# One level of Strassen's algorithm in a three-stage fused kernel: seven products of half blocks in place of eight, over chunks of 768 tokens

## The chip, the cores and the metric

The kernel runs on one core of one Trainium2 chip. The metric is device microseconds of one execution. The engines named below are PE (TensorE, matrix products), DVE (VectorE), ACT (ScalarE), POOL (GpSimd) and SP (SyncE, which here only issues DMAs). Each works through its own list of instructions in order and waits for others by counting semaphores.

## The reference, cut to what matters

Three stages follow each other, with fixed sizes: batch 4, 8 heads, 576 positions, head width 64; so 2304 tokens of width 512.

```python
# stage 0: two attentions per head, added (one on positions averaged by 4, one over |i-j| < 4)
x = (up(sm_attn(q_d, k_d, v_d)) + local_attn(q, k, v))      # 2304 x 512
# stage 1
xn = x / sqrt(mean(x*x) + 1e-6) * rms_g
y  = (silu(xn @ w_gate) * (xn @ w_val)) @ w_out             # 512 -> 1536 -> 512
# stage 2
h  = x @ w_in ; r = maximum(h, 0) ; out = (r*r) @ w_out     # 512 -> 2048 -> 512
```

Stage 1 has three matrix products (gate, value, output), stage 2 has two ("first" and "second").

## The kernel before, in words

**Precision.** Every matrix product of stages 1 and 2 is done in three passes of a 4-byte format (fp32r): each operand is split into a high part (a rounded copy, made on ACT) and a low part (the rest, a subtraction on DVE or POOL), and high x high, low x high and high x low are added in PSUM (`PASSES`). So one product of a 128-row weight block costs three matmuls per 128 rows of contraction.

**Stage 0** is 52 units `g` of attention (four groups of 13: nine "local" and four "down" units). For each unit PE forms scores (`qk`), DVE takes maxima, subtracts and sums, ACT takes exponents, POOL multiplies by the reciprocal sums (`normalise`), PE transposes and multiplies by v, ACT copies the output to `xT`, which holds the activations with the width on partitions. PE runs three to four units behind. POOL adds the "down" result at the end of a group (`add_down`). Into this phase other work is put by tables of unit numbers: the split of six weight pieces (`SPLIT_AT`), and for the first token chunk the squares, their sums and the twelve steps of the reciprocal root (`SQUARES_AT`, `SUM_SQ_AT`, `ROOT_AT`). After the last unit DVE normalises the first chunk and splits it (lines 760 and 766), and only then PE starts gate of chunk 0 (line 986).

**Stage 1** goes over six chunks of 384 tokens, and in each over 12 blocks `j` of 128 hidden columns. For each block PE does gate and value (`hidden`, line 986: 12 matmuls with a moving operand of 384 columns each) and the output product (`project`, line 1017: 12 matmuls of 384 columns into four PSUM banks). ACT takes the sigmoid from PSUM (line 540), DVE multiplies by gate and value out of PSUM (795, 798), ACT and DVE split the result (545, 802). The next chunk's mean square, root, normalisation and split are spread over the blocks. The activations `xs` have two buffers.

**Stage 2** goes over six chunks of 384 and 16 blocks `m` of 128: 12 matmuls of 384 columns (line 986 again), relu on ACT (605), square on DVE (840), split (610, 846), and the second product (`project2`, line 1085: 9 matmuls of 512 columns into three banks).

**Weights.** All of stage 1's weights lie split in SBUF: 36 pieces of 128x512, loaded once, with a high half made on ACT (line 495) and a low half on POOL (line 419). Stage 2's pieces take their places as stage 1's last chunk frees them. SP issues those loads in order of pieces (line 364).

PSUM has eight banks: four take the output product, two gate, one value, one the mean square (stage 1); two take the first product and six the second (stage 2). What orders the work is the order written out by hand for each engine. In the profile, lines of helpers are those of the copy `kernel.py`.

Of the kernel before, what the change touches and what calls it, by code (L numbers as in the profile page):

```python
# [48 lines left out]
C1 = 384  # L49
N1 = T // C1  # L50
C2 = 384
N2 = T // C2
TT2 = C2 // 128
PIECE = 512
NPIECE1 = 3 * J1
NPIECE2 = 2 * J2
PA = 6
NRAW = NPIECE1 + NPIECE2
FREE_0, FREE_1 = PA + 9, PA + 13
RING = 4  # L60
GSLOT = NPIECE2
LAG2 = 2
GRING = 4


SPLIT_AT = (21, 24, 27, 30, 35, 38)
SQUARES_AT = (34, 35, 37)
SUM_SQ_AT = (36, 37, 39)
MEAN_SQ_AT = 41
ROOT_AT = (42, 43, 44, 45, 46, 47, 48, 48, 49, 49, 50, 50)  # L70
# [5 lines left out]
ADD_DOWN_AT = (5, 7, 11, 12)  # L76
ADD_DOWN_OF = (0, 2, 1, 3)


def fused_kernel(nc, q_d, k_d, v_d, w1_d, w2_d, rms_d, out_d):  # L80
# [9 lines left out]
    with ctx:  # L90
# [8 lines left out]
        wrawA = [sb(f"wrawA{n}", [128, 2, PIECE], stack=rawA) for n in range(PA)]  # L99
        rawA.close()  # L100
        wsplitA = sb("wsplitA", [128, PA, 2, PIECE], f32r)
        gvec = sb("gvec", [128, KT])
        work = sb("work", [128, TT2 * DM])
        ssq, nrm, tmp = (work[:, C1 * x:C1 * x + C1] for x in range(3))
        ostage = work[:, :].rearrange("p (a b) -> p a b", a=TT2)
        xs0 = sb("xs0", [128, 2, KT, C1], f32r)
        ones = sb("ones", [128, 128])
# [8 lines left out]
        vquad = sb("vquad", [HK, 2, 2, FACTOR, GC], stack=att)  # L116
        qs[1] = sb("qs1", [128, NH, S], stack=att)
        kp[1] = sb("kp1", [128, NH, S + 2 * HALO], stack=att)
        vwin[1] = sb("vwin1", [KW, 2, NL, GC], stack=att)
        vd = sb("vd", [HK, 2, 2, GC], stack=att)  # L120
        qd = sb("qd", [128, NH, SDP], stack=att)
        kd = sb("kd", [128, NH, SD], stack=att)
# [10 lines left out]
        mask = sb("mask", [128, 3, KW], bf16, stack=att)  # L133
        identb = sb("identb", [128, 128], bf16, stack=att)
        ident = sb("ident", [128, 128], stack=att)
        att.close()

        rawB = ExitStack()
        wrawB = [sb(f"wrawB{n}", [128, 2, PIECE], stack=rawB) for n in range(NPIECE1 - PA)]
        rawB.close()  # L140
        wsplitB = sb("wsplitB", [128, NPIECE1 - PA, 2, PIECE], f32r)
        xs = [xs0, sb("xs1", [128, 2, KT, C1], f32r)]
        hb = sb("hb", [128, 2, 2, C1], f32r)
        sig = sb("sig", [128, 2, C1])
        prod = sb("prod", [128, 2, C1])

        def wslot(n):
            return wsplitA[:, n] if n < PA else wsplitB[:, n - PA]

        def wraw(n):  # L150
            return (wrawA[n] if n < PA else wrawB[n - PA])[:, 1, :]

        def slot_of(n):

            return n if n < NPIECE1 else n - NPIECE1

# [4 lines left out]
        ACC, G, V, SS = P[0:4], P[4:6], P[6], P[7]  # L161
        HID, OUT = P[6:8], [P[0:3], P[3:6]]
# [9 lines left out]
        wraw_in = [sem(f"wraw_in{i}") for i in range(RING)]  # L172
# [17 lines left out]
        wh_done, wl_done = sem("wh_done"), sem("wl_done")  # L190

        sq_done, ss_add, ss_mm, nr = sem("sq_done"), sem("ss_add"), sem("ss_mm"), sem("nr")
        xn_done, xh_done, xl_done = sem("xn_done"), sem("xh_done"), sem("xl_done")

        g_done, v_done, o_done = sem("g_done"), sem("v_done"), sem("o_done")
        sig_done, u_done, a_done = sem("sig_done"), sem("u_done"), sem("a_done")
        h_done, l_done = sem("h_done"), sem("l_done")
        y_done = sem("y_done")

        h2_done, o2_done = sem("h2_done"), sem("o2_done")  # L200
        r_done, s_done, gh_done, gl_done = sem("r_done"), sem("s_done"), sem("gh_done"), sem("gl_done")
        zh_done, zl_done = sem("zh_done"), sem("zl_done")
        ev_done = sem("ev_done")
# [8 lines left out]
        def number(eng, n):  # L212

            if not isinstance(n, int):
                eng.compute_val(n)
            return n

        def apart(eng):

            eng.wait_ge(consts, NCONST)  # L220
# [67 lines left out]
        def _(sp):  # L288
# [31 lines left out]

            load_k(0, K_PARTS[0], K_PARTS[1], k_part[0])
# [7 lines left out]
            for b in range(1, NG):  # L329
# [12 lines left out]
                if b == 1:  # L342
                    sp.dma_start(gvec[:, :], rms_d).then_inc(misc_in, 16)
                    for n in range(RING):
                        sp.dma_start(wraw(n), w1_d[n]).then_inc(wraw_in[n], 16)
                if b == 2:
                    for n in range(RING, PA):
                        sp.wait_ge(wh_done, n - RING + 1)
                        sp.dma_start(wraw(n), w1_d[n]).then_inc(wraw_in[n % RING], 16)

            for n in range(PA, NRAW):
                sp.wait_ge(wh_done, n - RING + 1)
                if n == PA:
# [785 lines left out]
```

## Time and profile before

| | |
|---|---|
| median of 3 runs | 1017.39 us (1017.31 to 1018.33) |
| profiled execution, its own time | 1024.89 us |
| its span (first to last instruction) | 1022.9 us |
| PE busy | 989.4 us (97%) |
| DVE, ACT, POOL busy | 423.8, 322.0, 162.9 us |
| mean granted TensorE clock | 0.973 of 2.4 GHz |

"PE" are matmuls and "PEld" the loads of their stationary operand; each matmul has one load. Both are pipelined: a matmul's recorded duration is longer than the distance to the next, so costs are read as distances (a count in a window where PE never idles), not as durations. A row of a group gives lines, engine, operation, tiles, shapes, the count, then busy time and mean ns of one, then the idle time ahead and what ended it.

### The profile page before, as it was taken

Reading aid. Unit: us, or ns where it says so; the run is one execution under the profiler, and the core shown is the slowest. Engines: PE = TensorE matmul, PEld = TensorE weight load, DVE = VectorE, ACT = ScalarE, POOL = GpSimd, SP = SyncE. Lnnn points to the kernel's source line nnn. Section 1 sums busy time; section 2 is a strip of 40 time slices with the busy share of each in tenths; the row PEclk is TensorE's granted clock in tenths of the full one; section 3 lists DMA queues with packets and bytes.
Section 4 is the critical chain, followed back from the end, with each engine's and each line's share of the span. In section 5 each row is a group of like instructions: output and inputs, shape, how many; then the busy total and the mean of one; then the engine's idle time right before and its main releaser. Section 6 shows DMA issues by size and latency. Waiting matters only on the chain.

```text
span 1022.9 us, 16131 instructions
## 1 busy us (share of the span) xinstructions
PE 989.4 (97%) x6404; PEld 918.7 (90%) x6404; DVE 423.8 (41%) x783; ACT 322.0 (31%) x698; POOL 162.9 (16%) x151
## 2 busy tenths in 40 slices
PE   6899959999999999999999999999999999999998
PEld 5677748999999999999999999999999999999997
DVE  6678892543443443443442322323333233332322
ACT  3556554442122122122123333223222222232221
POOL 3356556640000000000002661000000000000000
PEclk9779878999999999999999999999999999999999
DMA  9968302310000000000002440000000000000000
GB/s 241 175 149 211 89 2 93 123 53 1 1 1 1 1 1 1 1 1 1 1 1 64 133 133 2 1 1 32 1 31 1 1 31 1 16 16 1 31 1 31
DMA packets 27972, 42.84 MB, mean 42 GB/s; under 512 B 2300, under 2 KB 14972, under 8 KB 27516
## 3 DMA queue, kind: packets, MB, share of 16 engines
q1 hardware_dynamic: 26316, 40.64, 14.7%
q10 hardware_dynamic: 1584, 1.18, 0.4%
q8 instruction: 52, 0.85, 0.4%
q14 instruction: 20, 0.16, 0.1%
HBM read 37.10 MB, written 4.72 MB: 41 GB/s over the span
## 4 chain that ended last, share of the span: by engine, by line
PE 90%; DVE 5%; issue 3%; DMA 1%; ACT 1%; POOL 1%; SPq 0%; DVEq 0%; ACTq 0%
PE bank L986 49%; PE bank L1085 20%; PE bank L1017 15%; PE bank L922 1%; PE bank L941 1%; PE bank L962 1%; PE bank L916 1%; DVE sml L683 1%; PE bank L937 1%; PE bank L973 1%; DVE mxl L662 1%; DMA kp<-k_dram 1%; DVE qd L705 1%; PE bank L911 0%; PE bank L885 0%
## 5 line engine op out<-in xcount | busy, mean ns | idle before, releaser
L986 PE MATMUL bank<-xs,wsplitB 128*128 128x384 f32 x2376 | 436.8, 335 | 0.0
L986 PEld LDWEIGHTS bank<-xs,wsplitB 128*128 128x128 f32 x2376 | 416.8, 188 | 6.9
L1085 PE MATMUL bank<-wsplitB 128*128 128x512 f32 x702 | 174.4, 393 | 0.0
L1085 PEld LDWEIGHTS bank<-wsplitB 128*128 128x128 f32 x702 | 130.7, 188 | 23.7
L840 DVE TENSOR_TENSOR prod<-sig 128x384 f32<-128x384 f32 x96 | 53.6, 558 | 222.2 <-ACT sig L605 222.2
L1017 PE MATMUL bank<-hb,wsplitB 128*128 128x384 f32 x720 | 136.1, 336 | 1.4 <-ACT hb L545 1.4
L1017 PEld LDWEIGHTS bank<-hb,wsplitB 128*128 128x128 f32 x720 | 125.6, 188 | 3.3 <-POOL wsplitB L419 1.6
L798 DVE TENSOR_TENSOR prod<-prod,bank 128x384 f32<-128x384 f32 x72 | 39.9, 554 | 192.5 <-PE bank L986 192.4
L605 ACT ACTIVATE sig<-bank 128x384 f32<-128x384 f32 x96 | 47.2, 492 | 229.5 <-PE bank L986 229.5
L545 ACT CAST hb<-prod 128x384 fp32r<-128x384 f32 x72 | 37.0, 514 | 248.1 <-DVE prod L798 248.1
L986 PE MATMUL bank<-xs,wsplitA 128*128 128x384 f32 x504 | 96.4, 343 | 3.8 <-DVE xs L766 3.8
L986 PEld LDWEIGHTS bank<-xs,wsplitA 128*128 128x128 f32 x504 | 90.6, 191 | 6.0 <-issue 4.6
L419 POOL TENSOR_TENSOR wsplitB<-wrawB,wsplitB 128x512 fp32r<-128x512 f32 x56 | 72.8, 1327 | 35.3 <-ACT wsplitB L495 35.3
L846 DVE TENSOR_TENSOR wsplitB<-prod,wsplitB 128x384 fp32r<-128x384 f32 x96 | 53.6, 558 | 55.7 <-ACT wsplitB L610 55.7
L419 POOL TENSOR_TENSOR wsplitA<-wrawA,wsplitA 128x512 fp32r<-128x512 f32 x12 | 15.2, 1280 | 334.5 <-ACT wsplitA L495 334.5
L610 ACT CAST wsplitB<-prod 128x384 fp32r<-128x384 f32 x96 | 49.3, 514 | 60.0 <-DVE prod L840 60.0
L802 DVE TENSOR_TENSOR hb<-prod,hb 128x384 fp32r<-128x384 f32 x72 | 41.2, 572 | 42.2 <-ACT hb L545 42.2
L540 ACT ACTIVATE sig<-bank 128x384 f32<-128x384 f32 x72 | 35.5, 492 | 62.8 <-PE bank L986 62.8
L795 DVE TENSOR_TENSOR prod<-sig,bank 128x384 f32<-128x384 f32 x72 | 39.6, 550 | 27.8 <-ACT sig L540 27.8
L1085 PE MATMUL bank<-wsplitA,wsplitB 128*128 128x512 f32 x162 | 40.5, 394 | 0.0
L1085 PEld LDWEIGHTS bank<-wsplitA,wsplitB 128*128 128x128 f32 x162 | 30.2, 188 | 5.5
L962 PEld LDWEIGHTS bank<-probT,vwin 70*64 70x64 f32 x576 | 23.0, 155 | 10.9 <-issue 9.7
(75 smaller groups left out, 746.4 us busy)
## 6 DMA issues: line engine op xcount, KB each, us to landing
wrawB<-w_dram SPq DMA_DIRECT2D x56, 256.0 KB, 3.0
vquad<-v_dram SPq DMA_DIRECT2D x16, 288.0 KB
out_dram<-work SPq DMA_DIRECT2D x18, 256.0 KB, 2.0
kp<-k_dram SPq DMA_DIRECT2D x3, 1152.0 KB, 13.7
qs<-q_dram SPq DMA_DIRECT2D x3, 1152.0 KB, 20.8
vwin<-v_dram SPq DMA_DIRECT2D x6, 512.0 KB
wrawA<-w_dram SPq DMA_DIRECT2D x12, 256.0 KB, 4.7
vwin<-v_dram SPq DMA_DIRECT2D x2, 320.0 KB
```

What stands on the lines that cost most here:

```text
L419: nc.gpsimd.tensor_tensor(wslot(slot)[:, 1], wraw(slot), wslot(slot)[:, 0].bitcast(fp32), ALU.subtract).then_inc(wl_done, 1)
L545: nc.scalar.copy(hb[:, tp, 0, :], prod[:, tp, :]).then_inc(h_done, 1)
L605: nc.scalar.activation(sig[:, tp, 0:C2], HID[tp][:, 0:C2], ACT.Relu).then_inc(r_done, 1)
L610: nc.scalar.copy(wslot(GSLOT + gp)[:, 0, 0:C2], prod[:, tp, 0:C2]).then_inc(gh_done, 1)
L795: nc.vector.tensor_tensor(prod[:, tp, :], sig[:, tp, :], G[tp][:, 0:C1], ALU.mult).then_inc(u_done, 1)
L798: nc.vector.tensor_tensor(prod[:, tp, :], prod[:, tp, :], V[:, 0:C1], ALU.mult).then_inc(a_done, 1)
L802: nc.vector.tensor_tensor(hb[:, tp, 1, :], prod[:, tp, :], hb[:, tp, 0, :].bitcast(fp32), ALU.subtract).then_inc(l_done, 1)
L840: nc.vector.tensor_tensor(prod[:, tp, 0:C2], sig[:, tp, 0:C2], sig[:, tp, 0:C2], ALU.mult).then_inc(s_done, 1)
L846: nc.vector.tensor_tensor(w[:, 1, 0:C2], prod[:, tp, 0:C2], w[:, 0, 0:C2].bitcast(fp32), ALU.subtract).then_inc(gl_done, 1)
L986: last = mm(bank[:, 0:cols], wslot(n)[:, pw, 128 * k:128 * k + 128], x[:, px, k, 0:cols], start=(i == 0 and k == 0), stop=(i == 2 and k == ...
L1017: last = mm(ACC[m][:, 0:C1], wslot(3 * j + 2)[:, pw, 128 * m:128 * m + 128], hb[:, j % 2, px, :], start=(j == 0 and i == 0), stop=(j == J1 ...
L1085: last = mm(OUT[par][tt][:, :], gs[:, px, 128 * tt:128 * tt + 128], w[:, pw, :], start=(m == 0 and i == 0), stop=(m == J2 - 1 and i == 2))
```

## The change

Gate and value (and, in stage 2, the first products of two blocks of 128 columns) are one matrix product of 512 x 256 x 768 per block `u`. Over chunks of 768 tokens this product is cut in two along each of its three sides: contraction (2 x 256), hidden columns (2 x 128; gate and value, or two blocks of stage 2) and tokens (2 x 384). One level of Strassen's algorithm, in Winograd's form, gives the four quarter results from seven products (`NP = 7`) of combined operands instead of eight. Each product is 6 matmuls of 384 columns (`product`). There are 60 units: 3 chunks x 12, then 3 chunks x 8.

- The combined activations (`xcomb`, four sums, `combine_x`) and seven split operands `xs` (single buffer) are made per chunk: 7 copies on ACT (`x_high`) and 7 subtractions on DVE (`x_low`), each 768 elements per partition, and 4 combinations (POOL for the first chunk, DVE for the rest).
- The weights are no longer kept: each unit's four raw quarters are loaded again (4 DMAs of 128 KB), POOL makes four combinations (`combine`), ACT seven high parts (`weights_high`) and POOL five and DVE two low parts (`weights_low`), each 256 elements, one unit ahead, in two slots. Only the output weights stay (`wo`), loaded in order from the end of stage 0 on, behind a wait for all of stage 0.
- The results are summed out of two PSUM banks used in turn (`XY`): per unit ACT copies products 0 and 2 (`first_copy`, `copy_11`), DVE adds products 1, 3, 4, 5, 6 (`add`), each 384 elements.
- Sigmoid, gating and split then work from SBUF on 768 elements. The relu is folded with the square into one DVE instruction per 768 elements (`square`).
- The output product takes 24 matmuls per unit: 12 of 512 columns and 12 of 256 (`project`, 6 banks), cut into segments between the seven products and two units behind (`SEGS`, `LAG_P`). The second product of stage 2 takes 36 matmuls of 512 columns per unit, one unit behind (`SEGS2`).
- In the diff below the loops are, in this order, those of SP, POOL, DVE and PE.
- For the first chunk the mean square is taken with tokens on partitions: twelve root steps on 6 elements each, then spread by a diagonal (`diagonals` on POOL, `spread`), and normalisation and splits go into units 45 to 52 of the attention. For the other two chunks the root steps have 768 elements.

```diff
+HC = 384
+CS = 2 * HC
+U1, U2 = J1, J2 // 2
+BLK = 256
+NP = 7
+CONTINUES = (2, 5, 6)
+HIGH_ORDER = (0, 2, 5, 1, 3, 4, 6)
+POOL_LOW = (0, 2, 5, 1, 3)
+DVE_LOW = (4, 6)
+LAG_P = 2
+SEGS = (3, 3, 4, 3, 4, 3, 4)
+SEGS_FIRST = (0, 0, 4, 5, 5, 5, 5)
+SEGS2 = (0, 0, 5, 7, 8, 8, 8)
...
+        XY = [P[7], P[4]]
+        ACC = P[0:4] + P[5:7]
...
+            for u in range(NUF):
+                if u == 0:
+
+                    sp.wait_ge(oe_done, G_ALL)
                     sp.wait_ge(x_done, ND * NG)
+                    for n in range(3):
+                        load_wo(n)
+                if u < U1 - 3:
+                    load_wo(u + 3)
...
+                if u + 2 < NUF:
+                    load_w(u + 2)
...
+            for u in range(1, NUF - 1):
+                for n in range(4):
+                    combine(u + 1, n)
+                for p in POOL_LOW:
+                    weights_low(u + 1, p)
...
+            ROOT_PLACE = {5: (1, 2), 6: (3, 4, 5), 7: (6, 7, 8), 8: (9, 10, 11)}
+            NORM_PLACE = {9: (0, 1, 2, 3)}
...
+                add(u, 1)
+                if 0 < u <= NU1:
+                    gated(u - 1)
+                    valued(u - 1)
...
+                add(u, 3)
+                if 0 < u <= NU1:
+                    hidden_low(u - 1)
...
+                if normed:
+                    for n in ROOT_PLACE.get(j, ()):
+                        root(c + 1, n)
+                add(u, 4)
+                if prepares:
+                    weights_low(w, DVE_LOW[0])
...
+                if normed:
+                    for k in NORM_PLACE.get(j, ()):
+                        normalise(c + 1, k)
...
+                add(u, 5)
...
+            def product(u, p):
+                low_ready(pe, u, p)
+                if place(u) == 0:
+                    pe.wait_ge(xl_done, NP * chunk_of(u) + p + 1)
+                s = slot0(u) + p
+                bank_free(s)
                 for i, (pw, px) in enumerate(PASSES):
+                    for k in range(2):
+                        last = mm(XY[s % 2][:, 0:HC], wst[:, u % 2, p, pw, 128 * k:128 * k + 128], xs[:, p, px, k, :],
+                                  start=(p not in CONTINUES and i == 0 and k == 0), stop=(i == 2 and k == 1),
+                                  skip_group_check=True)
+                last.then_inc(pr_done, 1)
...
+            for u in range(NUF):
+                for p in range(NP):
+                    if u > 0 or p > 2:
+                        product(u, p)
...
+                    elif LAG_P <= u < NU1:
+                        n1 = n + (SEGS_FIRST if j == 2 else SEGS)[p]
+                        project(u - LAG_P, n, n1)
```

## Rows read from the trace of the kernel before

**Rows 1.** The page, busy time by engine and the span in 40 slices.
```profile
PE 989.4 (97%) x6404; PEld 918.7 (90%) x6404; DVE 423.8 (41%) x783; ACT 322.0 (31%) x698; POOL 162.9 (16%) x151
PEclk9779878999999999999999999999999999999999
GB/s 241 175 149 211 89 2 93 123 53 1 1 1 1 1 1 1 1 1 1 1 1 64 133 133 2 1 1 32 1 31 1 1 31 1 16 16 1 31 1 31
```
**Rows 2.** Chain that ended last, its shares by engine.
```profile
PE 90%; DVE 5%; issue 3%; DMA 1%; ACT 1%; POOL 1%; SPq 0%; DVEq 0%; ACTq 0%
```
**Rows 3.** Windows: stretch: its us, then each engine's busy us (instructions), clock, DMA.
```profile
350.00:450.00 100.00, 100.00 (x576) 99.73 (x575) 41.93 (x79) 21.23 (x43) 0.00 (x0) 1.00 0.00 1
800.00:900.00 100.00, 100.00 (x504) 90.67 (x503) 30.64 (x53) 26.43 (x51) 0.00 (x0) 1.00 0.05 17
120.00:135.00 15.00, 12.37 (x229) 9.85 (x230) 14.62 (x33) 7.35 (x20) 6.43 (x8) 1.00 0.01 3
135.00:147.00 12.00, 6.74 (x88) 5.06 (x86) 11.76 (x21) 6.79 (x23) 8.27 (x5) 0.81 0.01 1
```
**Rows 4.** Groups by line, whole span, PE and its weight loads.
```profile
L986 PE MATMUL bank<-xs,wsplitB 128*128 128x384 f32 x2376 | 436.8, 335 | 0.0
L986 PEld LDWEIGHTS bank<-xs,wsplitB 128*128 128x128 f32 x2376 | 416.8, 188 | 6.9
L1085 PE MATMUL bank<-wsplitB 128*128 128x512 f32 x702 | 174.4, 393 | 0.0
```
**Rows 5.** Timeline, start and length in us: a run of 64-column loads at full clock.
```profile
129.02 0.55 PEld L962 LDWEIGHTS bank<-probT,vwin 70*64 70x64 f32 x16 [0.20 <-issue]
```
**Rows 6.** Groups by line, DVE, 160 to 1022 us.
```profile
L840 DVE TENSOR_TENSOR prod<-sig 128x384 f32<-128x384 f32 x96 | 53.6, 558 | 222.2 <-ACT sig L605 222.2
L795 DVE TENSOR_TENSOR prod<-sig,bank 128x384 f32<-128x384 f32 x72 | 39.6, 550 | 27.8 <-ACT sig L540 27.8
L766 DVE TENSOR_TENSOR xs<-xT,xs 128x768 fp32r<-128x768 f32 x10 | 9.5, 953 | 0.0
```
**Rows 7.** Groups by line, POOL, whole span.
```profile
L419 POOL TENSOR_TENSOR wsplitB<-wrawB,wsplitB 128x512 fp32r<-128x512 f32 x56 | 72.8, 1327 | 35.3 <-ACT wsplitB L495 35.3
```
**Rows 8.** Timeline, DVE beside a busy POOL.
```profile
169.89 10.69 POOL L419 TENSOR_TENSOR wsplitB<-wrawB,wsplitB 128x512 fp32r<-128x512 f32 x8
173.15 0.94 DVE L802 TENSOR_TENSOR hb<-prod,hb 128x384 fp32r<-128x384 f32 x1 [0.95 <-ACT hb L545]
179.81 1.18 DVE L802 TENSOR_TENSOR hb<-prod,hb 128x384 fp32r<-128x384 f32 x1 [0.58 <-ACT hb L545]
```
**Rows 9.** Groups by line, DVE, 90 to 147 us: a root step and the smallest operation.
```profile
L745 DVE SCALAR_TENSOR_TENSOR work<-work 128x384 f32<-128x384 f32 x3 | 2.6, 864 | 0.0
L685 DVE RECIPROCAL sml<-sml 128x4 f32<-128x4 f32 x13 | 2.3, 178 | 0.4
```
**Rows 10.** Timeline at the start of stage 1.
```profile
146.95 2.10 DVE L760 SCALAR_TENSOR_TENSOR xT<-xT,gvec,work 128x384 f32<-128x384 f32 x2
149.03 1.23 PE L973 MATMUL bank<-pdT,vd 72*64 72x144 f32 x8
154.08 4.18 PE L986 MATMUL bank<-xs,wsplitA 128*128 128x384 f32 x12 [3.82 <-DVE xs L766]
163.55 5.13 POOL L413 TENSOR_TENSOR xT<-xT,outd 128x576 f32<-128x576 f32 x4 [13.73 <-ACT outd L490]
```
**Rows 11.** Page, DMA issues: KB each, us from issue to landing.
```profile
wrawB<-w_dram SPq DMA_DIRECT2D x56, 256.0 KB, 3.0
```
**Rows 12.** Groups by line, ACT, 160 to 1022 us.
```profile
L495 ACT CAST wsplitB<-wrawB 128x512 fp32r<-128x512 f32 x56 | 31.0, 619 | 2.0 <-DMA wrawB<-w_dram 2.0
L515 ACT CAST xs<-xT 128x768 fp32r<-128x768 f32 x10 | 8.3, 826 | 0.0
```
**Rows 13.** Timeline of the end.
```profile
1018.30 0.59 ACT L617 COPY work<-bank 128x512 f32<-128x512 f32 x1 [4.53 <-PE bank L1085]
1018.92 1.29 DVE L852 COPY work<-bank 128x512 f32<-128x512 f32 x2 [4.56 <-ACT work L617]
```

More of the change, by code:

```diff
@@ L140, in fused_kernel @@
         rawB.close()
[L141 to L155, printed above, removed]
+        late = ExitStack()
@@ new lines, in fused_kernel, with chunk_of, place, last_place @@
+        sb("pad1", [128, J1, 2, PIECE], stack=late)
+        hb += [sb(f"hb{n}", [128, 2, CS], f32r, stack=late) for n in (1, 2)]
+        late.close()
+        wo = sb("wo", [128, J2, 2, PIECE], f32r)
+        def chunk_of(u):
+            return u // U1 if u < NU1 else N1 + (u - NU1) // U2
+        def place(u):
+            return u % U1 if u < NU1 else (u - NU1) % U2
+        def last_place(u):
+            return U1 - 1 if u < NU1 else U2 - 1
+        def first_unit(q):
+            return U1 * q if q < N1 else NU1 + U2 * (q - N1)
@@ new lines, in summing, with slot0, slots, part @@
+        def summing(u):
+            return u < NU1 and place(u) == SS_UNIT and chunk_of(u) + 1 < N1
+        def slot0(u):
+            return NP * u + 2 * sum(summing(w) for w in range(u))
+        def slots(q):
+            return slice(CS * (q % N1), CS * (q % N1) + CS)
+        def part(q, d, h):
+            t0 = CS * (q % N1) + HC * h
+            return xT[:, 2 * d:2 * d + 2, t0:t0 + HC]
+        def x_source(q, p):
+            return (part(q, 0, 0), xcomb[:, 1], part(q, 1, 0), xcomb[:, 2], xcomb[:, 0], xcomb[:, 3],
+                    part(q, 1, 1))[p]
@@ L630, in _, with copy_11 @@
-            for t in range(LAG2):
-                relu(t, t % 2)
-                g_high(t, t % 2, t % GRING)
-            chunk2(0, 0, first=True)
-            chunk2(1, 1, prev0=True)
-            with act.Fori(1, N2 // 2 - 1) as cc:
-                chunk2(2 * cc, 0)
-                chunk2(2 * cc + 1, 1)
-            chunk2(N2 - 2, 0)
-            chunk2(N2 - 1, 1, last=True)
-            keep_out(N2 - 1, 1, False)
+                if g == G_ALL + 2:
+                    first_copy(0)
+            def copy_11(u):
+                act.wait_ge(pr_done, NP * u + 3)
+                if u <= NU1:
+                    ready(act, u_done, u)
+                else:
+                    act.wait_ge(r_done, 2 * (u - NU1))
+                nc.scalar.copy(gt[:, 0:HC], XY[slot0(u) % 2][:, 0:HC]).then_inc(cp_done, 1)
@@ new lines, in sigmoid, with hidden_high @@
+            def sigmoid(u, half):
+                if half == 0:
+                    act.wait_ge(cp_done, 2 * u + 2)
+                else:
+                    act.wait_ge(add_done, 5 * u + 5)
+                ready(act, u_done, u)
+                h = slice(HC * half, HC * half + HC)
+                nc.scalar.activation(sig[:, h], gt[:, h], ACT.Sigmoid).then_inc(sig_done, 1)
+            def hidden_high(u):
+                act.wait_ge(a_done, u + 1)
+                if u >= HRING:
+                    projected(act, u - HRING)
+                if u == 1:
+                    act.wait_ge(x_done, ND * NG)
+                nc.scalar.copy(hb[u % HRING][:, 0, :], prod[:, :]).then_inc(h_done, 1)
```

1036 lines of the change are left out of this document (623 added, 413 removed).

## The prediction

> **What bounds the kernel now.** I read the page first: PE is busy 97% of the span, DVE 41%, and the slices show the clock at full from 170 us on [rows 1]. The chain that ended last is 90% PE [rows 2]. The windows say what a matmul costs: in 100 us without a pause PE does 576 matmuls of 384 columns, so 0.1736 us each; in stage 2, 504 in 100 us, of which 288 have 384 columns and 216 have 512 (12 to 9), so (100 - 288 x 0.1736)/216 = 0.2315 us for 512 [rows 3]. The loops give 2880 matmuls on line 986 (6 chunks x (12 x 24 + 16 x 12); [rows 4] shows the 2376 of them whose weights lie in `wsplitB`), 864 on line 1017 and 864 on line 1085 (702 in [rows 4]): 500.0 + 150.0 + 200.0 = 850.0 us. Stage 1's first matmul starts at 154.08 and the last output copy at 1018.30 [rows 10, 13]: 864.2 us, so only 14.2 are not this stream. Stages 1 and 2 are bound by the number and length of matmuls. Stage 0's second half is bound by DVE: 14.62 of 15 us, then 11.76 of 12 [rows 3].
>
> **Part 1: matmuls.** The seven products give 60 x 42 = 2520 matmuls of 384 columns, 437.5 us instead of 500.0. The second product keeps its 864 of 512 columns, 200.0. The output product keeps its columns but turns 864 of 384 into 432 of 512 (100.0 us) and 432 of 256. The trace has no 256-column matmul with a 128-column load. From below: cost by columns, 0.1736 x 256/384 = 0.116 us. From above: 0.1736, if what sets the pace at 384 columns is the load and not the columns. A row speaks for the lower end: 16 loads of 64 columns, in two halves of the array side by side, fit in 0.55 us, the last one's own length (some 0.14) included, so 0.41/7 = 0.059 us per 64 columns and 0.117 per 128 [rows 5]. A load can thus just hide behind 256 columns; I take 0.117: 50.5 us. Sum 437.5 + 200.0 + 100.0 + 50.5 = 788.0, a gain of 62.0 us (62.4 at 0.116, 37.6 at 0.1736).
>
> The Trainium skill bears on this, in TensorE: Matmul & The Clock Gate. In "What overlaps and what doesn't" it says that a weight load overlaps running matmuls only when their row groups differ; "LDWEIGHTS (loading the stationary operand)" gives columns/1.2 ns, so 107 ns for 128. An estimate by both pages' figures puts 0.107 us in the open behind each of the 432 short matmuls, about 42 us more than my term. This trace disagrees with the overlap rule at 384 columns: every matmul here loads the whole array, and 0.1736 us leaves no room for a load in series [rows 3].
>
> **Part 2: stage 0.** DVE sets its pace, so DVE work put in costs its length. Removed from the loop: three sums (about 2.0 us) and twelve root steps (0.864 the dearest kind beside POOL [rows 9], 0.55 alone; 8.8). Added: four low parts of weights of 256 elements (4 x 0.5 = 2.0), three sums of 768 (3.6), twelve steps on 6 elements at a small instruction's 0.178 plus a wait for itself [rows 9] (2.9), four normalisations of 768 (1.0 alone, like a split's 0.953 [rows 6], up to the 1.05 that each half of that size took in [rows 10], taken as 1.3 each, 5.2) and five of the seven splits (0.953 alone [rows 6], 1.2 beside POOL, 6.0). That is 19.7 against 10.8: the loop ends 9 us later. In return the serial tail goes, in which PE, done with its attention work at 150.26 (149.03 + 1.23), waited 3.82 us for `xs` [rows 10]: its first seven operands are ready. Net +5 us for the first product of stage 1. Bounds: -3 (the POOL and ACT slack takes it all in) to +12: POOL gets 14 quarter-block operations, the diagonal and four combinations of 768 at 2.0 (1.327/512 per element), while it is busy 8.27 of 12 us already [rows 3, 7].
>
> **Part 3: the start of stage 1.** All new weights wait behind stage 0. SP waits for the last `oe_done` and for the four additions of POOL, 5.13 us [rows 10]; then it issues four output pieces (1 MB) and only behind them the four quarters of unit 2. At the best rate of a slice, 241 GB/s [rows 1], 1.5 MB take 6.2 us, plus some 1.5 of the 3.0 to landing [rows 11]. With T the start of the first product, attention ends at about T+6.5, the additions at T+11.6, and the weights land at T+19.4. ACT copies in order: its high part of the first output piece waits to T+14.7 with `first_copy` of unit 1 behind it, and PE waits for that bank before product (1,2); unit 2's high parts wait to T+19.4 with `copy_11` behind them, and PE waits before product (1,4). I get unit 2's start at T+24.2, against T+17.1 for 14 products (14.6) and the last transposes and values (2.5): 7 us of stall (5 to 12; a gap like this was followed by half clock, as before 154 us [rows 1, 10]).
>
> **Part 4: bank waits in stage 1.** A unit of PE is 42 x 0.1736 + 12 x 0.2315 + 12 x 0.117 = 11.5 us. DVE's ordinary share is five adds of 384 from PSUM (0.55), three operations of 768 (0.95), two of 256 (0.42): 6.5 us. ACT: two copies and two sigmoids of 384 (about 0.5), one copy of 768 (0.826), seven of 256 (0.36, from 0.619 for 512): 5.4 [rows 12]. POOL: nine of 256 elements at about 0.66 [rows 7]: 5.9. All fit. But two banks give DVE only one product's time: the add of product 4 must be done when product 6 starts, 2.4 us after product 4 ends. In blocks 6, 7, 8 three root steps of 768 (2.9 us) stand between adds 3 and 4: add 4 ends 1.3 us late, with POOL beside it 1.8 [rows 8]. Four normalisations (4.1) stand before add 5 in block 9: 1.9 late. With block 5 (0.8) that is 8.1 per chunk, for two chunks 16. Chunk boundaries add up to 1.5 each (splits of `xs` between the adds): 4. At block 2 of chunks 1 and 2 the output product waits for three copies of ACT with `copy_11` and a sigmoid in front: 2.2 each, 4.4. Together 25 us; 8 if DVE catches up in between, 40 if every one of its SBUF operations in these blocks meets POOL as in [rows 8].
>
> **Part 5: the rest.** Entering stage 2: the last output product waits for its low part, 1.7, and the first second product for six copies of ACT, 2.5: 4.2. Stage 2's unit is 7.3 + 36 x 0.2315 = 15.6 us and leaves DVE room; boundaries 3. The last split before the final 36 matmuls 0.7. Four fp32 sums of squares of 384 columns at about 0.64: 2.6. The HBM traffic for reloaded weights, 0.5 MB per 11.5 us (46 GB/s), is far under the 241 seen, and is priced at nothing. The end: one DVE copy in place of two after the last matmul [rows 13], -0.7.
>
> **Sum.** After the first product: 2.5 + 7 + 25 + 4.2 + 3 + 0.7 + 2.6 = 45 us beside the stream, against 14.2 now: +31. Total -62.0 + 5 + 31 - 0.7 = -26.7 us. The profiled execution took 1024.89 (span 1022.9), 7.5 above the median of 1017.39; I take the difference to the median: 990.7, forecast 991.
>
> **Rivals.**
> - The short matmul costs what 384 columns cost. For it: no shorter distance with a full load stands in the trace, and a load's recorded length is 0.188 us [rows 4]. Against: rows 5. The gain falls by 432 x (0.1736 - 0.117) = 24.4 us: 1015. This is also where the skill's overlap rule above would lead in kind.
> - The small queues cost little: the ordering keeps DVE ahead, so stage 1's bank waits are 8 instead of 25 and stage 0 grows by 2. Then 991 - 17 - 3 = 971.
> - Slower: POOL beside DVE. A DVE operation of 384 elements in SBUF takes 0.558 alone and 0.94 to 1.18 while POOL works without a pause [rows 8]; reads of PSUM are not slowed. Stage 1 gives DVE 99 us of adds and about 212 us of SBUF work (36 x 3.7, 8 for output weights, 37 for the next chunks' norms, 33 for their combinations and splits), in 36 x 11.5 = 414 us. Lengthened by a factor f it needs 99 + 212f; added to the 25 us of local waits already priced, it undoes the forecast gain when this passes 414 + 25 + 27, so from f = 1.73. At f = 1.9 DVE needs 502, and the time is 991 + 502 - 439 = 1054, at 1.75 it is 1022. Against: POOL works half of the unit (5.9 of 11.5), and an instruction that meets it waits at most one short POOL operation.
> - The products don't fall: excluded by the count of instructions in the diff.
>
> **Numbers.** Forecast mechanism (980 to 1003) 0.50; short matmul at full price 0.18; little waiting 0.21; DVE slower 0.11. Range 968 to 1016: it leaves out most of the slower case and the far ends of the others. A change within 0.2% (2 us) can't be told from none. Faster: the first three but for the upper tail of the second, 0.85; same 0.03; slower 0.12.
>
> **What would show it.** PE near 2520 matmuls of 384 in line with `product`, at 0.174 each; the distance behind a 256-column matmul near 0.117 (0.174 for the first rival); the first product starting near 159 us; a gap of some 7 us in units 1 and 2 released by ACT; waits of PE on `add` in blocks 5 to 9 of chunks 0 and 1 of 1 to 2 us; POOL and ACT under 60% busy. I am wrong if the first product starts after 166 us, if DVE is busy over 90% in stage 1, or if waits appear in stage 2 in each unit.

## The result and the profile after

The changed kernel takes 1052.73 us (median of 4, 1042.91 to 1058.97) against 1017.86 for the kernel before on the same chip. One of the four runs, 1058.97, counts as a slow one; the other three have the median 1049.71 and give the ratio, 1.031 (95% interval 1.027 to 1.036), and all differences from the changed kernel below start from that median. It is slower by 31.9 us, where 26.7 less was forecast. Even these three spread over 13 us, so that what an edit gains against this kernel is known to about 5 us. Its profiled execution took 1055.75 us (span 1054.0); set against the forecast on the same footing (1024.89 - 26.7 = 998.2) the gap is 57.6 us.

The page after, first the busy time of each engine, then the granted clock and the chain's shares, as in [rows 1, 2]:

```profile
PE 971.4 (92%) x6056; PEld 867.4 (82%) x6056; DVE 694.6 (66%) x1013; ACT 437.7 (42%) x1029; POOL 599.8 (57%) x628
PEclk9676585899998999998999999999999999999999
PE 62%; DVE 11%; issue 4%; ACT 2%; POOL 0%; DMA 0%; DVEq 0%; ACTq 0%
```

PE still does most, but its share of the ending chain fell from 90% to 62%, and nine slices have a clock digit below 9, where the kernel before has five. Windows (us, then busy time and count of PE, PEld, DVE, ACT and POOL, granted clock, DMA share, GB/s) say where:

```profile
560.00:617.50 57.50, 57.50 (x332) 54.96 (x331) 34.10 (x50) 24.97 (x60) 39.85 (x46) 1.00 0.16 47
160.00:175.00 15.00, 12.57 (x114) 9.00 (x110) 14.22 (x18) 10.17 (x27) 15.00 (x8) 0.50 0.01 2
185.00:300.00 115.00, 102.43 (x544) 94.19 (x543) 78.50 (x102) 52.43 (x117) 77.62 (x76) 0.93 0.22 69
300.00:415.00 115.00, 103.68 (x562) 95.83 (x561) 86.20 (x112) 53.39 (x119) 78.14 (x77) 0.97 0.13 37
```

In the third chunk of stage 1 (first line), which has no next chunk to normalise, PE never stops and a block takes 11.5 us, as forecast. In the first two chunks (last two lines) 115 us, which hold 660 matmuls at that pace, hold 544 and 562. The second line is the end of stage 0: half clock, GpSimd busy without a pause, VectorE nearly so.

Which waits these are is shown by PE's waits (who waits, on whom: us in total, times, longest):

```profile
PE bank L1351 <- DVE vt L1077: 28.0, 16, 3.2
PE bank L1381 <- ACT xT L771: 4.3, 2, 2.2
PE bank L1381 <- DVE hb L1091: 3.9, 1, 3.9
PE bank L1351 <- ACT m L705: 3.4, 2, 3.1
PE bank L1406 <- ACT xT L771: 2.2, 1, 2.2
PE bank L1351 <- POOL wst L549: 1.3, 2, 0.8
```

L1351 is `product`, L1381 `project`, L1406 `project2`, L1077 `add`. The 16 waits of the first line are local bank waits as in Part 4. One of them, block 7 of the second chunk, in the timeline (start, length, instruction, idle time before it):

```profile
447.63 1.23 PE L1351 MATMUL bank<-xs,wst 128*128 128x384 f32 x6
448.67 1.50 DVE L952 TENSOR_TENSOR tmp<-nrm 128x768 f32<-128x768 f32 x1
449.40 1.21 PE L1351 MATMUL bank<-xs,wst 128*128 128x384 f32 x6
450.28 1.31 DVE L954 SCALAR_TENSOR_TENSOR tmp<-tmp,ssq 128x768 f32<-128x768 f32 x1
451.69 1.29 DVE L957 SCALAR_TENSOR_TENSOR nrm<-tmp,nrm 128x768 f32<-128x768 f32 x1
452.91 0.54 DVE L1077 TENSOR_TENSOR vt<-vt,bank 128x384 f32<-128x384 f32 x1
453.60 1.29 PE L1351 MATMUL bank<-xs,wst 128*128 128x384 f32 x6 [2.53 <-DVE vt L1077]
```

The first PE line is product 4, complete at 448.86. Its add stands on DVE behind three root steps in a row, from 448.67 to 452.98, and begins only at 452.91, 4.05 us after the product. PE makes product 5 in the other bank meanwhile; product 6 needs product 4's bank and starts at 453.60.

The other new loss lies in stage 0. SyncE's queue after:

```profile
46.83 0.44 SPq L417 DMA_DIRECT2D wraw<-w_dram  x1
70.41 0.33 SPq L411 DMA_DIRECT2D stage<-w_dram  x1
71.73 0.43 SPq L417 DMA_DIRECT2D wraw<-w_dram  x1
72.28 0.38 SPq L403 DMA_DIRECT2D kp<-k_dram  x1
72.70 0.51 SPq L450 DMA_DIRECT2D qs<-q_dram  x1
```

and the same two loads of the third head group in the kernel before:

```profile
46.58 0.40 SPq L319 DMA_DIRECT2D kp<-k_dram  x1
47.02 1.77 SPq L335 DMA_DIRECT2D qs<-q_dram  x1
```

The second `load_w` of the change waits, in its first line, for a low part that GpSimd makes in attention unit 23. SyncE stands at that wait from 47.3 to 70.41, with the keys and queries of group 2 behind it: they are issued 25.7 us late. PE and DVE run out of work:

```profile
81.85 0.44 PE L1258 MATMUL bank<-mask,identb 64*64 64x280 bf16 x2 [9.06 <-issue]
83.26 0.45 DVE L876 TENSOR_REDUCE mxl<-bank 128x4 f32<-128x280 f32 x1 [9.92 <-PE bank L1263]
```

Attention unit 26 begins 5.6 us later than before, unit 38 20.4, unit 51 30.8, and stage 1's first product starts at 181.06, not at 154.08 [rows 10]. The delay grows behind the gap while PE is at half clock: by the clock records from 67.1 to 94.4, 104.7 to 132.0, 142.2 to 145.6 and 155.9 to 186.6 us, where in the kernel before it is so from 63.9 to 77.6, 101.5 to 111.7 and 142.4 to 159.5. In these stretches PE sets the pace: units 27 to 29 follow each other at 3.9 us, where before it was 2.1, and in the second window here PE never stops while DVE has room:

```profile
80.00:100.00 20.00, 18.15 (x210) 13.95 (x212) 10.81 (x24) 7.77 (x20) 4.94 (x7) 0.64 1.10 216
115.00:130.00 15.00, 15.00 (x128) 11.89 (x125) 9.29 (x17) 6.93 (x22) 8.48 (x6) 0.50 0.00 1
```

The gap did not bring the first of them about: the clock had fallen at 67.1, behind a wait of 1.3 us for `prob`, and the gap began at 72.8.

### The profile page after: what moved, and what is told of

Same layout as the page of the kernel before. It is cut to its first block, busy times and chain, and to the rows that moved or that the text cites. A ratio compares the mean times of both kernels' runs of the same rounds, so it can differ in the third digit from the quotient of the medians.

```text
span 1054.0 us, 17656 instructions
## 1 busy us (share of the span) xinstructions
PE 971.4 (92%) x6056; PEld 867.4 (82%) x6056; DVE 694.6 (66%) x1013; ACT 437.7 (42%) x1029; POOL 599.8 (57%) x628
## 4 chain that ended last, share of the span: by engine, by line
PE 62%; DVE 11%; issue 4%; ACT 2%; POOL 0%; DMA 0%; DVEq 0%; ACTq 0%
PE bank L1351 34%; PE bank L1406 19%; PE bank L1381 10%; DVE prod L1087 1%; DVE xs L1010 1%; DVE prod L1083 1%; DVE vt L1077 1%; DVE xT L990 1%; DVE tmp L952 1%; DVE tmp L954 1%; ACT xs L697 1%; DVE wst L1017 1%; ACT hb L755 1%; ACT wst L662 0%; DVE xcomb L1006 0%
## 5 line engine op out<-in xcount | busy, mean ns | idle before, releaser
L1351 PE MATMUL bank<-xs,wst 128*128 128x384 f32 x2520 | 514.9, 344 | 34.7 <-DVE vt L1077 28.0
L1351 PEld LDWEIGHTS bank<-xs,wst 128*128 128x128 f32 x2520 | 450.6, 192 | 63.0 <-issue 42.3
L549 POOL TENSOR_TENSOR wst<-wraw,wst 128x256 fp32r<-128x256 f32 x240 | 227.3, 966 | 203.5 <-ACT wst L662 203.0
L1406 PE MATMUL bank<-wo,gs 128*128 128x512 f32 x864 | 218.4, 393 | 2.9 <-ACT xT L771 2.2
L1381 PE MATMUL bank<-hb,wo 128*128 128x512 f32 x864 | 193.6, 342 | 8.2 <-ACT xT L771 4.3
L1406 PEld LDWEIGHTS bank<-wo,gs 128*128 128x128 f32 x864 | 160.3, 188 | 31.3 <-DVE wo L1118 2.5
L1381 PEld LDWEIGHTS bank<-hb,wo 128*128 128x128 f32 x864 | 149.8, 193 | 17.8 <-issue 9.1
L1077 DVE TENSOR_TENSOR vt<-u,bank 128x384 f32<-128x384 f32 x120 | 66.1, 551 | 100.3 <-PE bank L1351 100.0
L662 ACT CAST wst<-wraw 128x256 fp32r<-128x256 f32 x360 | 123.7, 408 | 8.6 <-DMA wraw<-w_dram 5.0
L1077 DVE TENSOR_TENSOR u<-m,bank 128x384 f32<-128x384 f32 x60 | 33.2, 553 | 108.3 <-PE bank L1351 99.9
L532 POOL TENSOR_TENSOR wraw<-wraw,stage 128x256 f32<-128x256 f32 x60 | 57.5, 959 | 79.0 <-DMA wraw<-w_dram 74.0
L543 POOL TENSOR_TENSOR wraw<-wraw 128x256 f32<-128x256 f32 x60 | 51.9, 864 | 36.4 <-PE bank L1351 36.4
L549 POOL TENSOR_TENSOR wst<-stage,wst 128x256 fp32r<-128x256 f32 x60 | 69.2, 1153 | 0.0
L1077 DVE TENSOR_TENSOR vt<-vt,bank 128x384 f32<-128x384 f32 x60 | 33.1, 552 | 48.8 <-PE bank L1351 47.7
L536 POOL TENSOR_TENSOR wraw<-wraw 128x256 f32<-128x256 f32 x60 | 57.2, 954 | 4.5
L538 POOL TENSOR_TENSOR wraw<-wraw 128x256 f32<-128x256 f32 x60 | 57.3, 955 | 0.0
## 6 DMA issues: line engine op xcount, KB each, us to landing
kp<-k_dram SPq DMA_DIRECT2D x3, 1152.0 KB, 15.4
```

The lines of the kernel that those rows point to most:

```text
L532: nc.gpsimd.tensor_tensor(block[4], block[3], stage[:, :], ALU.add).then_inc(wc_done, 1)
L536: nc.gpsimd.tensor_tensor(block[1], block[4], block[0], ALU.subtract).then_inc(wc_done, 1)
L538: nc.gpsimd.tensor_tensor(block[3], block[0], block[3], ALU.subtract).then_inc(wc_done, 1)
L543: nc.gpsimd.tensor_tensor(block[6], block[2], block[1], ALU.subtract).then_inc(wc_done, 1)
L549: nc.gpsimd.tensor_tensor(b[:, 1, :], w_source(w, p), b[:, 0, :].bitcast(fp32), ALU.subtract).then_inc(wlp_done, 1)
L662: nc.scalar.copy(wst[:, s, p, 0, :], w_source(w, p)).then_inc(wh_done, 1)
```

## The experiments

Beside each time stand three sums read from its trace. T is the start of stage 1's first product. Waits and half clock come from the distances between the starts of neighbouring matmuls behind T: what a distance has over the full-clock one (0.1736, 0.2315 and 0.117 us for 384, 512 and 256 columns) is a wait if it is 0.01 us or more, except in half-clock stretches, where up to 0.320, 0.427 and 0.213 is booked as half clock and only the rest as wait. The sums of squares are left out.

| kernel | median us (runs) | ratio to before [95%] | T | waits | half clock |
|---|---|---|---|---|---|
| changed | 1049.7 (3) | 1.031 [1.027, 1.036] | 181.1 | 55.8 | 15.4 |
| e1_queue | 1037.8 (4) | 1.020 [1.017, 1.022] | 164.2 | 54.3 | 16.5 |
| e9_norm_spread | 1010.4 (8) | 0.994 [0.992, 0.996] | 162.7 | 32.9 | 7.5 |
| e5_norm_by_token | 1006.5 (4) | 0.988 [0.986, 0.990] | 165.3 | 28.4 | 9.0 |
| e6_order | 993.9 (4) | 0.977 [0.975, 0.978] | 164.8 | 18.1 | 4.5 |
| e7_start | 987.2 (4) | 0.971 [0.968, 0.975] | 163.9 | 16.2 | 1.6 |

**e1_queue**: the second early weight load goes behind group 2's keys and queries.

```diff
                     load_w(0)
-                    load_w(1)
...
                 sp.dma_start(qs[b % 2][:, :, :], rows_of(q_d, b, 0, S)).then_inc(q_in[b], 16)
+                if b == 2:
+                    load_w(1)
```

> The changed kernel with one edit: unit 1's four weight quarters are asked for after the q and k of head group 2 instead of ahead of them. Theory (SyncE's order plus the clock): the wait of SyncE for POOL's low part in attention unit 23 kept group 2's q and k back, PE stood 9.1 us, and stage 0 then ran behind a TensorE at half clock. Without it attention unit 26 starts near 75 to 78 us instead of 83, and stage 1's first product near 160 to 165 us instead of 181; the time falls by 15 to 22 us, to about 1033. Rival (the gap is absorbed): stage 0 is bound by DVE later on, so the first product moves by under 5 us and the time by no more.

1037.81 us: 11.9 less, a little under what was expected. Queries go out at 47.28, the gap of 9 us is gone, T is 164.25, 16.8 earlier, and the bank waits are the same (28.5 us in 16). The clock falls here too, at 67.2, but is full again at 74.1, not at 94.4. The shift of T is no accident of one trace: the four kernels with SyncE's order as changed have it at 178.0 to 185.3 (e10_norm_by_token_alone, e2_no_norm and e3_pool_aside besides the changed one), the five with this order and all of chunk 0's work at 162.7 to 165.3. So one wait in a queue of an idle engine cost some 12 us.

```profile
47.28 1.47 SPq L450 DMA_DIRECT2D qs<-q_dram  x1
70.21 0.33 SPq L411 DMA_DIRECT2D stage<-w_dram  x1
72.33 0.44 PE L1259 MATMUL bank<-mask,identb 64*64 64x280 bf16 x2
```

**e4_before_late_load**: the same lateness put into the kernel before, with nothing else of the change.

```diff
             for b in range(1, NG):
+                if b == 2:
+                    sp.wait_ge(qk_done, 25)
```

> The kernel before with one wait added: SyncE asks for group 2's q and k only when the scores of attention unit 24 are done, about 70 us. Theory (the late load alone does it): attention unit 26 starts near 82 us instead of 77.7, with a PE gap of 5 to 9 us and half clock behind it, and stage 1 starts 8 to 16 us later; the time is 1026 to 1034. Rival (absorbed by DVE's pace later): under 4 us.

1025.91 us, 7.8 more (ratio 1.008, 1.006 to 1.011), at the low edge. Late loads of group 2 alone cost time. Here the keys go out at 65.99 and PE stands 5.6 us; in the changed kernel they went out at 72.28, PE stood 9.1, and the order cost about half as much again. In the traces the first gate matmul comes only 1.8 us later, not the 8 to 16 that I expected, but the trace of the kernel before is a poor measure here: PE is at half clock in it from 63.9 to 77.6 us, and the three units from 22 on take 11.2 us there and 6.2 in this run, before the gap.

**e2_no_norm**: the changed kernel, with the root steps and normalisations of chunks 1 and 2 on 8 of 768 columns; it leaves the rest of these two chunks unnormalised.

```diff
-                root_step(n, ssq[:, :], tmp[:, :], nrm[:, :], nr, 11 * (q - 1) - 1)
+                root_step(n, ssq[:, 0:8], tmp[:, 0:8], nrm[:, 0:8], nr, 11 * (q - 1) - 1)
```

> The changed kernel with the root steps and normalisations of chunks 1 and 2 cut from 768 to 8 elements (the rest of those chunks is left unnormalised, so this part of the computation is left out); counts and waits stay. Theory (bank waits): in blocks 5 to 9 of chunks 0 and 1 PE waits for adds that stand behind this DVE work, 1 to 3.5 us each. Those waits (12.5 us in chunk 0, 13 in chunk 1) and the half clock behind them (5 and 4 us) go; stage 1 from first product to unit 36 takes about 440 us instead of 474, the time falls by 25 to 33 us. Rival (POOL beside DVE in general): waits come from DVE being slow everywhere; then blocks 5 to 9 keep over 1 us each and the time falls by under 12 us.

1027.17 us, 22.5 less than the changed kernel. PE's waits on `add` for `vt` fall from 28.0 us in 16 to 7.7 in 11, the longest from 3.2 to 1.1. Behind the first product the trace has 21.2 us less of waits and 9.6 less of half clock; the first product itself comes 4.3 later, in a stage that the edit does not touch. The norm's wide operations make most of the local waits.

**e3_pool_aside**: GpSimd holds its weight work back while the root steps run.

```diff
             for u in range(1, NUF - 1):
+                if normed_place(u - 1):
+                    pool.wait_ge(add_done, 5 * (u - 1) + 4)
                 for n in range(4):
                     combine(u + 1, n)
                 for p in POOL_LOW:
+                    if normed_place(u) and p == 1:
+                        pool.wait_ge(add_done, 5 * u + 3)
                     weights_low(u + 1, p)
```

> The changed kernel, same work, but in blocks 5 to 9 of chunks 0 and 1 POOL holds back its weight work until DVE is through its root steps (after add 4) or normalisations (after add 5). Theory (POOL beside DVE costs): root steps and normalisations fall from 1.3 to 1.5 us back to 0.96, the wait before product 6 in blocks 6 to 8 from 2.8 to about 1.5 us and that before block 10 from 3.5 to about 1.8; together 9 to 12 us less, 12 to 15 with the clock. Rival (it is the amount of DVE work alone, or POOL then comes late): the waits stay above 2.3 us, or new waits of PE for weights appear, and the time falls by under 4 us or rises.

1038.03 us, 11.7 less, of which the first product's start may give 3.1 (an accident of stage 0). In the trace waits fall by 9.0 us and half clock by 4.9; the waits of blocks 6 to 8 fall from 2.7 each to 1.5 to 2.4. Groups of DVE from 180 to 640 us (line, operation, count | busy, mean ns), in the changed kernel and then here:

```profile
L952 DVE TENSOR_TENSOR tmp<-nrm 128x768 f32<-128x768 f32 x6 | 9.0, 1496 | 0.0
L954 DVE SCALAR_TENSOR_TENSOR tmp<-tmp,ssq 128x768 f32<-128x768 f32 x6 | 7.8, 1304 | 0.6
L957 DVE SCALAR_TENSOR_TENSOR nrm<-tmp,nrm 128x768 f32<-128x768 f32 x6 | 7.7, 1290 | 0.6
```

```profile
L959 DVE TENSOR_TENSOR tmp<-nrm 128x768 f32<-128x768 f32 x6 | 6.2, 1041 | 0.0
L961 DVE SCALAR_TENSOR_TENSOR tmp<-tmp,ssq 128x768 f32<-128x768 f32 x6 | 5.8, 959 | 0.6
L964 DVE SCALAR_TENSOR_TENSOR nrm<-tmp,nrm 128x768 f32<-128x768 f32 x6 | 5.8, 959 | 0.6
```

The same step takes 0.959 with GpSimd aside and 1.30 beside it: three in a row are 1.1 us longer, about what the waits had over the forecast of 1.8. The adds, which read PSUM, take 0.55 in both. The Trainium skill has this in SBUF — State Buffer, "SBUF: two separate sides": a VectorE instruction with two SBUF inputs and a GpSimd instruction that reads SBUF exclude each other for the whole of the one that came first. The rows agree in kind: 0.959 and 1.30 for two SBUF inputs, 0.55 and 0.55 with one from PSUM.

**e9_norm_spread**: e1_queue with all the wide norm work kept, one operation per gap between adds instead of three and four in a row.

```diff
-            ROOT_PLACE = {5: (1, 2), 6: (3, 4, 5), 7: (6, 7, 8), 8: (9, 10, 11)}
-            NORM_PLACE = {9: (0, 1, 2, 3)}
+            NORM_WORK = {      # (block, after how many of its adds)
+                (3, 3): [(sum_squares, 0)], (4, 0): [(sum_squares, 1)], (4, 3): [(sum_squares, 2)],
+                (5, 3): [(root, 1)], (5, 4): [(root, 2)],
+                (6, 0): [(root, 3)], (6, 3): [(root, 4)], (6, 4): [(root, 5)],
...
+                (9, 0): [(normalise, 0)], (9, 3): [(normalise, 1)],
+                (9, 4): [(normalise, 2)], (10, 0): [(normalise, 3)],
```

> e1_queue (1037.8) with the norm of chunks 1 and 2 as wide as before, nothing taken away, but its 11 root steps and 4 normalisations stand one at a time: after add 5's and add 4's place and before add 1, over blocks 5 to 10, where the changed kernel has three steps in a row ahead of add 4 and four normalisations ahead of add 5. It tells placing from amount. My theory (local order: each gap between two adds leaves 1.65 us of slack-free time, which a single step of 1.3 plus a low part of 0.5 fills but does not overrun by much): the waits of blocks 6, 7, 8 and 10 (2.8, 2.8, 2.8, 3.5) fall to 1 or less each, and the time by 12 to 20 us, to 1018 to 1026. Rival (VectorE has too much work in these blocks, as in the forecast's slower case): lateness adds up from gap to gap, the waits return at another bank, and the time falls by less than 5.

1010.35 us: 27.5 less than e1_queue, more than I expected, and below the kernel before. Its page's busy times, and PE's waits on `add` for `vt` (28.5 us in 16 in e1_queue):

```profile
PE 950.4 (95%) x6056; PEld 851.5 (85%) x6056; DVE 694.2 (69%) x1013; ACT 438.0 (44%) x1029; POOL 608.7 (61%) x628
```

```profile
PE bank L1360 <- DVE vt L1078: 3.6, 4, 1.1
```

DVE is busy 694.2 us, as in e1_queue (694.2), in as many instructions; only their order differs. The lateness did not add up from gap to gap: DVE always had the time, not at that place. This settles the rival of a full DVE.

**e5_norm_by_token**: the kernel of e1_queue, in which chunks 1 and 2 get their inverse root as chunk 0 does: the sums by token, 12 steps on 6 elements, a diagonal by GpSimd, two spreading matmuls, four normalisations one at a time.

```diff
+                (5, 0): [(root, 0), (root, 1), (root, 2)], (5, 3): [(root, 3), (root, 4), (root, 5)],
+                (5, 4): [(root, 6), (root, 7), (root, 8)], (6, 0): [(root, 9), (root, 10), (root, 11)],
+                (8, 0): [(normalise, 0)], (8, 3): [(normalise, 1)],
+                (9, 0): [(normalise, 2)], (9, 3): [(normalise, 3)],
...
                 if summing(u):
-                    square_sums(chunk_of(u) + 1)
+                    token_sums(chunk_of(u) + 1)
+                if spreading(u):
+                    spread(chunk_of(u) + 1, 0)
+                    spread(chunk_of(u) + 1, 1)
```

> On top of e1_queue (1037.8): chunks 1 and 2 get their inverse root as chunk 0 does. PE sums the squares per token (six matmuls of one column), VectorE does its twelve steps on 6 elements, GpSimd builds the diagonal (768), PE spreads it (two matmuls of 384), ScalarE copies it out; the four normalisations of 768 stand singly in blocks 8 and 9. Nothing is left out. My theory (in-order VectorE work between two adds holds PE's banks, and the half clock follows the waits): leaving the norm's work out gave 25.5 us on the changed kernel; here some of it stays (four normalisations per chunk, spread), so 20 to 25 us less than e1_queue: 1013 to 1018; waits of blocks 6 to 8 fall from 2.8 to under 1. Rival (the gain of leaving it out came from less GpSimd contention or fewer instructions overall, and a wait only moves): 1025 or more, with new waits of 2 us in blocks 7 to 9 at the spread and the normalisations.

1006.54 us, 31.3 less than e1_queue, more than the 20 to 25 expected from e2_no_norm. That kernel still had its 22 root steps one behind the other, at 8 columns each, and four normalisations in a row. Against e9_norm_spread the small steps bring only 3.8 us.

**e10_norm_by_token_alone**: that norm on the changed kernel, SyncE's order left as it was.

```diff
-                root_step(n, ssq[:, :], tmp[:, :], nrm[:, :], nr, 11 * (q - 1) - 1)
+                root_step(n, rs[:, 0, 0:TT], rs[:, 1, 0:TT], rs[:, 2, 0:TT], nrc, 12 * q, source=bank[:, 0:TT])
```

> The changed kernel (1052.7) with the norm by token of e5_norm_by_token and nothing else, to see whether that gain stands by itself and adds to the queue's. Additive: 31 us less, 1021 to 1022, the first product still at 181. If the two gains overlap (the clock's half-speed stretches shared between them), 15 to 25 less, 1028 to 1038.

1021.28 us (10 runs; ratio 1.003, 1.000 to 1.006), 28.4 less, the first product at 182.6. With e1's 11.9 that makes 40.3; both together (e5_norm_by_token) gave 43.2. Within what is known of the changed kernel's time the two gains add up.

**e6_order**: e5, with four of the six copies of a finished chunk moved to the end of ScalarE's preceding block, and the last hidden low part ahead of the output weights.

```diff
+                if (j == 1 and first and c > 0) or u == NU1:
+                    for n in range(4):
+                        keep_y(c - 1, n)
...
+                if u == NU1:
+                    hidden_low(u - 1)
                 if follows:
                     x_low(c, 5)
                 add(u, 3)
```

> e5_norm_by_token, and the order of two places mended: ScalarE takes four of the six copies of the finished output chunk at the end of the block before (they stood in front of copy_11 in block 2 and of unit 37's squares), and VectorE puts the last hidden low part ahead of the second output weights on entering stage 2. My theory: waits of 2.4 us at block 2 of chunks 1 and 2, 4.2 at unit 36 and 2.4 at unit 37 go nearly whole, 8 to 10 us less than e5. Rival (PE then waits at the next bank in line): under 3 us less.

993.85 us, 12.7 less than e5_norm_by_token, more than expected. Waits fall by 10.3 us, half clock by 4.5; what is left at unit 36 is 2.0 (5.0 before), at unit 37 0.9 (2.4), at block 2 of the two chunks 0.4 (5.2 together).

**e7_start**: e6, and SyncE issues the weights of unit 2 before it waits for the end of attention; the first output high and low part move one block later.

```diff
+            load_w(2)
             for u in range(NUF):
                 if u == 0:
                     sp.wait_ge(oe_done, G_ALL)
...
-                if u < J1:
+                if 0 < u < J1:
                     second_high(u)
```

> e6_order, and the start of stage 1 mended: SyncE issues the weights of unit 2 before it waits for the end of stage 0 (the changed kernel issues them behind the four output pieces), and ScalarE's first output high part and VectorE's low part move one unit later. My theory: the waits of units 1 and 2 (6.5 us) and the half clock behind them (4.4) shrink to under 3 in all: 5 to 9 us less than e6, so about 1000 to 1005, below the kernel before. Rival: the unit's weights wait for GpSimd's four late additions, not for the queue: same as e6.

987.16 us, 6.7 less than e6_order, 2.9% below the kernel before (ratio 0.971, 0.968 to 0.975). From its page, and a window to set beside that of the changed kernel:

```profile
PE 941.5 (96%) x6080; PEld 846.6 (86%) x6080; DVE 678.7 (69%) x1011; ACT 438.4 (45%) x1033; POOL 591.7 (60%) x630
PEclk9798775999999999999999999999999999999999
```

```profile
185.00:300.00 115.00, 113.90 (x651) 107.64 (x650) 95.69 (x130) 57.37 (x132) 92.34 (x90) 1.00 0.21 63
```

The clock is full from the eighth slice (172 us) on, and the window that held 544 matmuls now holds 651.

**e8_stage0_norm_short**: e1_queue with chunk 0's four normalisations on 8 columns; it leaves the rest of chunk 0 unnormalised.

```diff
+                cols = 8 if q == 0 else CS
+                x = xT[:, k, CS * q:CS * q + cols]
```

> e1_queue with the four normalisations of chunk 0 on 8 of 768 columns (the rest of chunk 0 stays unnormalised); one profile, for the start of stage 1's first product, 164.25 us in e1_queue. If VectorE's added work sets the pace of stage 0's tail, the first product comes 4 x 1.2 = 5 us earlier, near 159.5. If GpSimd (14.4 of 15 us busy in 145 to 160) or the clock at half sets it, it stays within 1 us of 164.

The first product starts at 159.8, 4.4 us earlier (1032.06 us, one run). DVE sets the pace of stage 0's tail, as the forecast had it.

## Why the prediction was wrong

Terms of the forecast against the changed kernel's trace, in us:

| term | forecast | measured | difference |
|---|---|---|---|
| matmuls, Part 1 | 788.0 | 791.8 by the distances | +3.8 |
| first product starts, Part 2 | 159.1 | 181.1 | +22.0 |
| start waits, Part 3 | 7 | 6.5 | -0.5 |
| bank waits of stage 1, Part 4 | 25 | 41.0 | +16.0 |
| half clock behind the first product | 0 | 15.4 | +15.4 |
| entering stage 2, Part 5 | 4.2 | 7.4 | +3.2 |
| stage 2's boundaries and last split | 3.7 | 0.9 | -2.8 |
| sum | | | +57.1 of 57.6 |

Between the medians the gap is 58.7 (1049.7 against 991), since the two traced runs lie 7.5 and 6.0 us above theirs.

**Part 1 held.** In the window from 560 to 617.5 five blocks fill 57.5 us. Read one by one, the distances there average 0.1171 us behind the 60 matmuls of 256 columns (forecast 0.117), 0.2305 behind the 60 of 512 and 0.1751 behind the 210 of 384. Over the whole run those of `product` average 0.1755 and not 0.1736; with the others that makes the 3.8 us of the first row. The first rival, the short matmul at full price, is out. The runs also disagree with the rule of the Trainium skill (TensorE: Matmul & The Clock Gate, "What overlaps and what doesn't") that a load overlaps matmuls only where their row groups differ: here it lies hidden even behind 256 columns, at 0.117 us a pair.

**Part 2 is the step that failed first.** I counted DVE's added and removed operations in stage 0 and their 9 us. T of e1_queue (164.2) lies within my bounds of -3 to +12, and e8 shows that DVE's work counts there at nearly its length. I did not count the issuing queue. `load_w` begins with a wait on `low_ready`; I read its four DMAs as free since SyncE has nothing else to do. But behind it stood group 2's loads, and with them all attention. That is 16.8 of the 22 us, and some 12 us of the time (e1_queue). The other 5.2 are within the bounds; what they are made of no run separates. A first product after 166 us was named as what would prove the forecast wrong.

**Part 4 had the mechanism and missed its size.** The waits lie in the blocks named: 6, 7, 8 at 2.7 each (forecast 1.8), 10 at 3.4 (1.9, as block 9's lateness), 4 and 5 at 0.8 to 1.7. The norm's blocks have 28 us where I had 16, the chunk boundaries 7 where I had 4; block 2 of chunks 1 and 2 has 2.3 each, as forecast. The failed assumption is the price of three root steps, 2.9 alone and half a microsecond more beside GpSimd: their mean lengths add up to 4.1 (1.496, 1.304 and 1.290). I had the row for it, [rows 8], and took it whole only for my upper bound of 40, which is close to what came (41.0). GpSimd is busy 77.62 of 115 us, 67% and not the half that I worked out with 0.66 us for each of its operations. Of all 300 operations of L549, 47 meet no DVE instruction and take 0.73 us, and 150 that DVE covers for over nine tenths take 1.13 (line, form, count | busy, mean ns):

```profile
L549 POOL TENSOR_TENSOR wst<-wraw,wst 128x256 fp32r<-128x256 f32 x240 | 227.3, 966 | 203.5 <-ACT wst L662 203.0
L532 POOL TENSOR_TENSOR wraw<-wraw,stage 128x256 f32<-128x256 f32 x60 | 57.5, 959 | 79.0 <-DMA wraw<-w_dram 74.0
```

**The half clock was not priced at all.** I noted under Part 3 that a gap was followed by half clock, and then counted 25 us of waits at their own length. (The row that I gave for it is no such case: before 154.08 the clock had been at half since 142.4, and the gap began at 150.26.) Of the 15.4 us, 1.8 belong to the stretch of stage 0 that ends at 186.6. The rest lies in seven stretches, each behind one of the 13 waits of 2.3 to 4.1 us, with 1.2 to 2.6 us of loss each; six such waits had none behind them. In e7, with no single wait over 1.3 us, 1.6 us is left, all of it in the first block. Taken together, the waits cost 1.24 times their length (55.8 and 13.6).

**Part 3 held, and Part 5 in part.** PE waits 3.1 us on ACT's `m` before product 2 of unit 1 and 0.8 on its `gt` before product 4, where the forecast had them. Entering stage 2, the copies cost 2.4 (forecast 2.5), but the last output product waits 4.1 for its low part and not 1.7, because DVE makes low parts of output weights first; in e6 that wait is 1.1.

**The slower rival was priced from the wrong quantity.** It asked whether DVE's sum of work exceeds stage 1, with a factor of 1.73 as the point from which it decides. The factor is 1.36 to 1.57 (1.30 and 1.50 over 0.955), DVE is busy 292 of the 415 us from 185 to 600, 70%, and e9 shows the same work without the waits. That its 1054 at f = 1.9 lies beside the measured time is luck: its mechanism is not the one that ran. The range of 968 to 1016 left no room for queue, half clock and contention together.

The gain of 62 us in matmuls is there all the same: with its orders mended (e7_start) the kernel runs at 987.2, with a first product at 163.9 and 16.2 us of waits.

## What to carry to other kernels

Before a DMA is moved into an idle queue, read the first wait of the block that issues it and list what is queued behind: an idle engine's queue is the critical path once someone waits there. With two PSUM banks, an in-order engine's slack has to be had between each two adds, not on average; put helper work in one operation per gap, at the price it has beside GpSimd, before thinking about doing less of it. Then price every remaining wait of a few microseconds on TensorE with the half clock that may follow.

## What was not expected of the hardware

A two-input VectorE operation of 768 fp32 elements took 0.96 us alone and 1.3 to 1.5 beside GpSimd, while one reading PSUM stayed at 0.55. Waits as short as 2.3 us on a busy TensorE (block 2 of chunk 1 in e1_queue), once of 1.8 us (at 425.35 in e3_pool_aside, half clock from 425.6 to 429.0), were followed by stretches at the half clock level, in the changed kernel 13.6 us of loss; behind waits of 1.3 us and less there were none in e7's stage 1, after its first block. A full-array load of 128 columns hides behind a 256-column matmul at 0.117 us a pair. The traced run of the kernel before lies 7.5 us above its median; its attention units 22 to 24, mostly at half clock, take 5.0 us more than in e4_before_late_load, which may be the larger part. Why the clock fell there is open.
